# Output weights times Fourier table in three fp32r passes, with the weights' low part made by an accumulating DMA

## The reference

```python
# 1 attention with decaying state, per head
state = alpha[:, :, t, :, None] * state + einsum('bhd,bhe->bhde', k[:, :, t], v[:, :, t])
y[:, :, t] = einsum('bhd,bhde->bhe', q[:, :, t], state)
# 2 gated projection
gate = 1 / (1 + exp(-causal_conv5(x)))
x = (gate * (x @ w_val)) @ w_out
# 3 Fourier mixing, then a block of two matmuls
u = x + real(fft(fft(x, axis=1), axis=2))
un = (u - mean(u)) / sqrt(var(u) + 1e-6)
out = u + relu(un @ w_ch1) @ w_ch2
```

## Time and profile before

| | |
|---|---|
| median of 3 runs | 549.63 us (549.59 to 549.74) |
| profiled execution | 549.4 us |
| its span | 547.5 us |
| TensorE busy | 540.4 us |
| VectorE busy | 397.7 us |
| ScalarE busy | 207.6 us |
| stretch of the three `wd` products | 31.85 to 46.98 us |

### The profile page before, as it was taken

The page is one execution under the profiler, slowest core; times in us unless marked ns, Lnnn a source line. Parts: engine busy times, 40 slices in busy tenths (PEclk is TensorE's granted clock), DMA queues, the critical chain, the costliest instruction groups (busy, mean ns, idle before and its releaser), DMA issues.

```text
span 547.5 us, 13458 instructions
## 1 busy us (share of the span) xinstructions
PE 540.4 (99%) x5539; PEld 519.0 (95%) x5539; DVE 397.7 (73%) x874; ACT 207.6 (38%) x487; POOL 13.0 (2%) x29
## 2 busy tenths in 40 slices
PE   7999999999999999999999999999999999999997
PEld 7989999999999999999999999999999999999997
DVE  8998889999857786989767486998936484653322
ACT  5555554424352125325262134325244134322221
POOL 0010000000000000000000000000000000000000
PEclk9999999999999999999999999999999999999999
DMA  8878111453212010456322001256200000022000
GB/s 265 243 272 302 45 44 55 118 168 117 72 57 73 31 44 27 129 143 173 91 62 68 29 1 45 87 141 204 70 12 19 30 2 0 1 59 81 16 22 30
DMA packets 36302, 47.21 MB, mean 86 GB/s; under 512 B 11633, under 2 KB 25201, under 8 KB 35985
## 3 DMA queue, kind: packets, MB, share of 16 engines
q1 hardware_dynamic: 34080, 40.97, 25.3%
q0 software_dynamic: 1728, 5.11, 2.7%
q10 hardware_dynamic: 432, 0.27, 0.2%
HBM read 35.32 MB, written 11.01 MB: 85 GB/s over the span
## 4 chain that ended last, share of the span: by engine, by line
PE 93%; DVE 4%; issue 1%; DMA 1%; ACT 1%; SPq 0%; DVEq 0%
PE bank L1076 45%; PE bank L1165 28%; PE evens L1103 4%; PE bank L1150 4%; PE bank L1145 2%; PE bank L1233 2%; PE bank L1196 2%; PE sums L1127 2%; PE bank L1267 1%; PE bank L1202 1%; DMA a_in<-in_alpha_dram 1%; DVE w_lo L999 1%; PE bank L1277 1%; PE sums L1112 0%; DVE scores L960 0%
## 5 line engine op out<-in xcount | busy, mean ns | idle before, releaser
L1058 DVE SCALAR_TENSOR_TENSOR h_lo<-bank,h_hi 128x256 fp32r<-128x256 f32 x144 | 60.1, 418 | 94.2 <-ACT h_hi L795 89.8
L1076 PE MATMUL bank<-unT_hi,w_hi 128*128 128x256 f32 x432 | 123.7, 286 | 0.9 <-DVE h_lo L1058 0.6
L795 ACT ACTIVATE h_hi<-bank 128x256 fp32r<-128x256 f32 x144 | 55.0, 382 | 177.1 <-PE bank L1076 177.0
L1076 PE MATMUL bank<-unT_lo,w_hi 128*128 128x256 f32 x432 | 122.2, 283 | 0.0
L1076 PE MATMUL bank<-unT_hi,w_lo 128*128 128x256 f32 x432 | 121.3, 281 | 0.0
L1165 PE MATMUL bank<-w_hi,h_hi 128*128 128x384 f32 x288 | 98.8, 343 | 0.0
L1165 PE MATMUL bank<-w_lo,h_hi 128*128 128x384 f32 x288 | 97.6, 339 | 0.0
L1165 PE MATMUL bank<-w_hi,h_lo 128*128 128x384 f32 x288 | 97.3, 338 | 0.0
L1076 PEld LDWEIGHTS bank<-unT_hi,w_hi 128*128 128x128 f32 x432 | 81.2, 188 | 4.1 <-DVE h_lo L1058 1.7
L1076 PEld LDWEIGHTS bank<-unT_hi,w_lo 128*128 128x128 f32 x432 | 81.6, 189 | 0.0
L1076 PEld LDWEIGHTS bank<-unT_lo,w_hi 128*128 128x128 f32 x432 | 81.4, 189 | 0.0
(11 more groups left out here) (187 smaller groups left out, 958.0 us busy)
## 6 DMA issues: line engine op xcount, KB each, us to landing
v_in<-in_v_dram SPq DMA_DIRECT2D x24, 224.0 KB, 3.2
w_raw<-in_w_dram SPq DMA_DIRECT2D x2, 2304.0 KB, 10.3
a_in<-in_alpha_dram SPq DMA_DIRECT2D x44, 96.9 KB, 2.2
q_in<-in_q_dram SPq DMA_DIRECT2D x44, 96.0 KB, 2.2
k_in<-in_k_dram SPq DMA_DIRECT2D x44, 96.0 KB, 2.4
turned_blocks<-turned SPq DMA_DIRECT2D x15, 256.0 KB, 2.3
kdT<-turned_blocks SPq DMA_DIRECT2D x60, 64.0 KB, 2.0
out_dram<-u POOLq DMA_DIRECT2D x18, 192.0 KB, 2.3
```

Source lines behind the costliest of these rows:

```text
L795: act.activation(h_hi[:, f % HBUF, :], ps[:, 0:GW], ACT.Relu).then_inc(s_hi, 1)
L1058: dve.scalar_tensor_tensor(h_lo[:, f % HBUF, :], ps[:, 0:GW], 0.0, h_hi[:, f % HBUF, :].bitcast(F32), ALU.max, ALU.subtract).then_inc(s_re ...
L1076: last = pe.matmul(ps, l, r, start=(i == 0), stop=(i == len(mms) - 1))
```

## The change

`wd` is done like the other products, as three fp32r passes over three blocks: nine matmuls of 388 columns instead of three in full precision. The table comes from the host in two parts, `dft_hi` and `dft_lo`, loaded by POOL's DMAs once the second chunk's `inv` is done. The transposed weights are loaded by SP beside chunk 2 (`w_val` moves to chunk 4). Their parts are made in two new steps on ACT with one DMA between them. `thi` writes minus the weights, rounded to fp32r, to `woutT_hi`. POOL then issues a DMA that adds `woutT_hi` to `woutT`, so that the rounding error is left there. `tlo` copies that to `woutT_lo` and turns the sign of `woutT_hi` in place. `LATE` gets these steps and changes the order of `wd`, `wdl`, `tapj` and `whi` in chunks 3 and 4.

```diff
-LATE = {0: [("tapj", 0, 0, 0), ("odd", 0, 0, 0)], 1: [("tapj", 0, 1, 0)], 2: [("tapj", 0, 2, 0), ("whi", 0, 0, 0), *x_parts("xhi", 0)],
-        3: [("wd", 0, 0, 0), ("tapj", 0, 3, 0), ("wdl", 0, 0, 0), ("tapv", 0, 0, 1), ("xlo", 0, 0, 0), ("tapv", 0, 0, 2)],
-        4: [("wd", 0, 1, 0), ("tapj", 0, 4, 0), ("wdl", 0, 1, 0), ("tapv", 0, 0, 3), ("wlo", 0, 0, 0), ("tapv", 0, 0, 4)]
+LATE = {0: [("tapj", 0, 0, 0), ("odd", 0, 0, 0), ("thi", 0, 0, 0)], 1: [("tapj", 0, 1, 0)], 2: [("tapj", 0, 2, 0), ("tlo", 0, 0, 0), *x_parts("xhi", 0)],
+        3: [("tapj", 0, 3, 0), ("wd", 0, 0, 0), ("whi", 0, 0, 0), ("tapv", 0, 0, 1), ("xlo", 0, 0, 0), ("tapv", 0, 0, 2)],
+        4: [("wdl", 0, 0, 0), ("wd", 0, 1, 0), ("tapj", 0, 4, 0), ("wdl", 0, 1, 0), ("tapv", 0, 0, 3), ("wlo", 0, 0, 0), ("tapv", 0, 0, 4)]
...
-            beside = {2: ("wval",), 3: ("dft",), 4: ("woutT",), 5: ("wout", "w1", "w2")}
+            beside = {2: ("woutT",), 4: ("wval",), 5: ("wout", "w1", "w2")}
...
+            pool.wait_ge(s_inv, 2)
+            for dst, part_ in ((dft_hi, 0), (dft_lo, 1)):
+                pool.dma_start(dst[:, :, :], dft_d[part_]).then_inc(s_dload, 16)
+            pool.wait_ge(s_thi, 1)
+            pool.dma_start(woutT[:, :, :], woutT_hi[:, :, :].bitcast(F32), accum_op=ALU.add).then_inc(s_tadd, 16)
             pool.wait_ge(s_xc, NCH - 1)
...
+                elif kind == "thi":
+                    act.wait_ge(s_tload, 16)
+                    act.activation(woutT_hi[:, :, :], woutT[:, :, :], ACT.Copy, scale=-1.0).then_inc(s_thi, 1)
+                elif kind == "tlo":
+                    act.wait_ge(s_tadd, 16)
+                    act.activation(woutT_lo[:, :, :], woutT[:, :, :], ACT.Copy)
+                    act.activation(woutT_hi[:, :, :], woutT_hi[:, :, :].bitcast(F32), ACT.Copy, scale=-1.0).then_inc(s_tlo, 1)
...
                 elif kind == "wd":
                     pe.wait_ge(s_dload, 32)
-                    for k_ in range(K):
-                        last = pe.matmul(ps[:, 0:2 * NC], woutT[:, k_, cols], dftd[:, k_, :],
-                                         start=(k_ == 0), stop=(k_ == K - 1))
-                    last.then_inc(s_unit, 1)
+                    pe.wait_ge(s_tlo, 1)
+                    product(ps[:, 0:2 * NC], [(woutT_hi[:, k_, cols], woutT_lo[:, k_, cols], dft_hi[:, k_, :],
+                                               dft_lo[:, k_, :]) for k_ in range(K)]).then_inc(s_unit, 1)
```

More of the change, by code:

```diff
@@ L299, in build @@
                 w_raw[name] = at(name + "_raw", [128, K, n], F32, lo)
+        TB, FB = K * D * 4, (K * 2 * NC * 4 + 31) // 32 * 32
         woutT = at("woutT", [128, K, D], F32, hi)
-        dftd = at("dftd", [128, K, 2 * NC], F32, hi + K * D * 4)
+        woutT_lo = at("woutT_lo", [128, K, D], F32R, hi)
+        woutT_hi = at("woutT_hi", [128, K, D], F32R, hi + TB)
+        dft_hi = at("dft_hi", [128, K, 2 * NC], F32R, hi + 2 * TB)
+        dft_lo = at("dft_lo", [128, K, 2 * NC], F32R, lo)
+        assert 2 * TB + FB <= K * FF * 4
         z1 = region(2 * FULLB)
@@ L441, in build @@
         s_dload = sem("dft_loaded")
+        s_tload = sem("transposed_wout_loaded")
+        s_thi = sem("transposed_wout_hi")
+        s_tlo = sem("transposed_wout_lo")
+        s_tadd = sem("transposed_wout_lo_added")
         s_small = sem("odd_tables_loaded")
@@ L574, in _ @@
                 for name in beside.get(c, ()):
[L575 to L578, removed]
+                    if name == "woutT":
+                        sp.dma_start(woutT[:, :, :], w_out_t).then_inc(s_tload, 16)
                     else:
@@ L1304, in two_parts @@
     high = (table.view(np.uint32) & np.uint32(0xFFFFF000)).view(np.float32)
-    return np.stack([by_rows(high, 256), by_rows(table - high, 256)])
+    return np.stack([by_rows(high, table.shape[1]), by_rows(table - high, table.shape[1])])
 def fourier_constants():
@@ L1323, in fourier_constants @@
     f = np.float32
-    return {"dft_d": by_rows(dft_d.astype(f), 2 * NC), "fold_cos": two_parts(cos[order][:, order[:256]].astype(f)),
+    return {"dft_d": two_parts(dft_d.astype(f)), "fold_cos": two_parts(cos[order][:, order[:256]].astype(f)),
             "fold_nsin": two_parts(nsin[order][:, order[:256]].astype(f)),
```

## The result

| kernel | median us | lowest to highest us | executions |
|---|---|---|---|
| before | 549.58 | 549.13 to 551.75 | 12 |
| changed | 551.34 | 550.24 to 553.98 | 12 |

The ratio is 1.0033, with an interval of 1.0025 to 1.0042: slower by 1.76 us. The forecast was 549.9 us, no change that can be measured. The time lies inside the range, but above 550.7 us, the bound that the prediction itself set for slower, to which it gave a chance of 0.20. Two things stand out before any row is read: the lowest times (550.24, 550.27) are 0.6 to 0.7 us above before, and the other ten spread over 3 us (550.95 to 553.98), where eleven of the twelve of before lie within 0.6 us (549.13 to 549.74). That suggests a constant cost of a few tenths, and a second one that changes from execution to execution.

A forecast was written before the change was run, and what follows sets the result against it. TensorE, busy 99% of the span, was taken as the bound. Two cheaper products (-0.72), the xT wait (+1.03) and woutT (+0.1), less up to 0.1, gave +0.3 us: 549.9 us, range 548.8 to 551.6.

The forecast's parts named there:

- Part 1: Matmuls of the three products: nine fp32r matmuls at 0.178 us, 1.60 us, so each product 0.36 us shorter.
- Rival D: Three passes cost as much as the full-precision product, +1.0 instead of +0.3: 550.6 us; chance 0.05.
- the sum: -0.72 (two products) + 1.03 (diagonals wait for xT) + 0.1 (woutT) = +0.4, less up to 0.1: +0.3 us.
- The third product: ACT is already late behind it: its 0.36 us is lost, wdl still starts 3.33 us after it.
- The gap of 0.6 us: Sign of a right forecast: a gap of about 0.6 us on TensorE before the third wdl.
- Part 2: ACT in chunk 2: one more 1.07 us pass delays the xT copy; TensorE waits 1.03 us at chunk 3's diagonals.
- Rival A: Clean gain: xT in time, all cost hidden, 0.72 to 1.1 us off, 548.5 to 548.9; chance 0.10.
- Part 3: ACT in chunk 0: thi adds 1.07 us; xT usable at 19.98, TensorE needs it at 20.02: hidden.
- Part 4: Loads: POOL's two early tables delay woutT, costing 0.1 us, range 0 to 0.9; alpha block's delay hidden.
- rival B: POOL's tables hold woutT past 18.1; 0.4 to 0.9 us more on TensorE: 550.3 to 550.8; chance 0.18.
- Part 5: Accumulating DMA takes 7 us, landing at 27, hidden from ACT; range 4 to 12, up to 3 us late.
- Rival C: Accumulating DMA lands after 28.78, holding up ACT and TensorE: 551.1 at 10 us, 553.1 at 12; chance 0.16.

## Why the prediction held where it did, and where it didn't

- **Part 1 held.** In the first profile of the changed kernel nine matmuls took 35.45 to 37.21 = 1.76 us in the first product (sixteen hundredths more than 9 x 0.178, at its two ends: 0.26 from its first row to the second, 0.27 from the last to the sums), 40.59 to 42.18 = 1.59 in the second. Rival D falls. The gain of both together, 0.61 us without any wait, is the 0.72 of the sum less its 0.1.
- **The third product** gave nothing, as forecast: its `wdl` starts 48.56 - 45.23 = 3.33 us after it. The gap of 0.6 us is there by starts (46.93 to 48.56 is 1.63 us, 1.03 without a wait); the idle time in the bracket, 0.36 us, counts from the modelled end of the matmuls and is shorter.
- **Part 2 held.** 1.03 us forecast at the diagonals; the starts 32.85 and 34.34 are 1.49 apart, 0.49 without a wait, so 1.00. Taking one pass away removed 0.74 of it. Rival A falls.
- **Part 3 held** in what it says of TensorE: in none of the profiled executions does it wait for `xT` at chunk 1's diagonals.
- **Part 4 failed, in its choice of what to look at.** It asked whether `woutT` would be late (it wasn't: landed after 5.6 us, rival B falls) and whether the alpha block would be, and priced the tables at 0.1 us. By the Trainium skill's rule of turns between queues ("DMA: Bandwidth & Descriptors", "Queues, rings and completion order") `woutT` would be hardly held up, and 5.6 us beside 5.8 for the load in its place before agrees. But SP's queue holds the chunks' loads too, and the one that TensorE came to wait for was `v_in`, which the working never named. The tables cost 0.6 us by themselves. The rows to see it were there: the share was already 1.03 from 11 to 14 us, so 1.19 MB more asked for at 10.5 us could only be moved over chunk 2's loads. The `v_in` of chunk 2 landed at 15.07 + 2.7 = 17.8 us before and its sums started at 22.34: 4.6 us to spare, and the landing of 7.9 us for a load issued at 15.76 ends at 23.7, past it. The alpha rows, which Part 4 counted as hidden, were waited for as well once the tables came a chunk later (1.73 us on VectorE, 0.97 us on TensorE).
- **Part 5 failed in the same way.** Its range of 4 to 12 us held, the 7 us taken was low (6.6, 10.4, 11.6, 9.7, 10.4, 6.9 and 9.3 us in the seven profiles that have it), and in four of seven it was in time for ACT. Rival C is real, but small: ACT waited in three of them, 0.3, 0.45 and 1.19 us. The step that failed is the word "hidden": the transfer was priced by who waits for it, not by whom it holds up. By that it costs some 0.8 us of the median with the tables early, and less with the loads spread. The Trainium skill's halved rate for an add ("Collectives: The Full Stack", "The bandwidth ceiling: the fold count and why AG ≠ RS ≠ AR"), stated there for collectives, gave 8.0 to 11.6 us as an estimate; five of seven landings agree, but a plain copy in its place took 7.3 us, so the trace can't say that the halved rate is what makes them long.
- **The sum** of +0.3 was right for the stretch it describes (0.34 in the trace), and even the fastest execution was 0.6 to 0.7 us above before. The missing term was some 1.4 us for the loads that Parts 4 and 5 made late, which turns "no change" into "slower".
- **That the range held is luck.** Its upper end, 551.6 us, was there for rival C, ACT held up by the accumulating DMA. C cost ACT 1.19 us at most and mostly nothing; the measured 551.34 us came about by loads that no rival named.

## What to carry to other kernels

Price a transfer twice: by when it lands for its own reader, and by what it does to every other load that is in flight or issued in the same stretch; where the DMA share is near 1 already, list all loads of the next chunks with the time each has to spare, and take the smallest. Waits in a row don't add: one that comes first can swallow the next, so a gain measured in one version of a kernel may be absent in another. A wait that one edit opens can be closed by moving the work to an idle engine: here the change is worth 0.5 us once GpSimd makes the low part and the loads are spread, and costs 1.8 us without that. A median that rises more than the lowest time does points to something that varies between executions, and one profile won't show all of it.

## What was unexpected of the hardware

- A DMA of 576 KB from on-chip memory to on-chip memory with adding landed after 6.6 to 11.6 us with other loads running; loads of 224 KB beside it took up to 10.8 us instead of 2.7.
- GpSimd subtracts 128x1152 elements in 2.63 us by the profile, whose spans on this engine are rough. VectorE's scan that starts beside it takes 2.05 us in all three profiles with the subtraction, 1.23 elsewhere; the scores before it (1.23 us) and the products after it (0.66, 0.68) keep their time. VectorE had the 0.8 us to spare here, since TensorE waited for nothing of it:

```profile
20.49 0.17 DVE L951 RECIPROCAL ends<-lam 128x4 f32<-128x4 f32 x1
20.70 2.05 DVE L953 TENSOR_TENSOR_SCAN kd<-a_in,ends 128x516 f32<-128x516 f32 x1
```

```profile
19.03 2.63 POOL L643 TENSOR_TENSOR woutT_lo<-woutT,woutT_hi 128x1152 fp32r<-128x1152 f32 x1 [2.02 <-ACT woutT_hi L712]
21.61 0.56 POOL L644 DMA_DIRECT2D dft_lo<-in_dft_d_dram  x1
```

- The granted clock fell to 0.50 for about 3.4 us early in two profiled executions, at a cost of some 1.4 us. Ahead of it TensorE was idle for 0.28, 0.78 and 0.75 us between 7 and 11.4 us in the changed kernel (0.28, 0.78 and 0.76 with GpSimd and early tables); but the plain-copy kernel had 0.71, 0.78 and 0.74 us there and kept the full clock, so these gaps alone don't decide it.
